# Score products of even and odd heads, alternating in one block behind both decay products

## The reference

```python
# for each step t
m_new = maximum(f + m, i);  f_stab = exp(f + m - m_new);  i_stab = exp(i - m_new)
C = f_stab * C + i_stab * outer(v, k);   n = f_stab * n + i_stab * k
y = sigmoid(o) * (C @ q) / maximum(abs(n . q), 1)
# layer 2: rms norm, then (silu(xn @ w_gate) * (xn @ w_val)) @ w_out     (320 -> 1536 -> 320)
# layer 3: g = h+ + alpha * h-  with h = x @ w_in;  g @ w_out2           (320 -> 2048 -> 320)
```

## Time and profile before

| | us |
|---|---|
| median of 3 runs | 541.23 (541.06 to 547.64) |
| span of the profiled execution | 539.5 |
| TensorE (PE) busy in it | 509.5 (94%) |
| VectorE (DVE) busy | 365.5 (68%) |
| ScalarE (ACT) busy | 203.3 (38%) |
| GpSimd (POOL) busy | 233.1 (43%) |

### The profile page before, as it was taken

The page is one execution under the profiler, slowest core; times in us unless marked ns, Lnnn a source line. Parts: engine busy times, 40 slices in busy tenths (PEclk is TensorE's granted clock), DMA queues, the critical chain, the costliest instruction groups (busy, mean ns, idle before and its releaser), DMA issues.

```text
span 539.5 us, 9907 instructions
## 1 busy us (share of the span) xinstructions
PE 509.5 (94%) x3113; PEld 485.2 (90%) x3113; DVE 365.5 (68%) x710; ACT 203.3 (38%) x508; POOL 233.1 (43%) x250
## 2 busy tenths in 40 slices
PE   5889888999999999999999999999999999998996
PEld 4778788998999999998999899999899899997996
DVE  7634589557899847346899848444999842228885
ACT  1322244434453532324453432324453432235452
POOL 3520066552564723423464723424374632223764
PEclk9755599999999999999899999999999999999999
DMA  7633742122333394000343477000333420003553
GB/s 129 162 63 49 148 134 78 50 70 47 73 111 107 83 143 68 1 1 24 66 124 88 105 119 95 0 0 0 76 108 106 103 73 2 0 1 77 129 140 97
DMA packets 80725, 41.14 MB, mean 76 GB/s; under 512 B 51548, under 2 KB 80684, under 8 KB 80684
## 3 DMA queue, kind: packets, MB, share of 16 engines
q1 hardware_dynamic: 80684, 40.65, 33.7%
HBM read 38.67 MB, written 1.97 MB: 75 GB/s over the span
## 4 chain that ended last, share of the span: by engine, by line
PE 41%; issue 25%; DVE 12%; POOL 12%; DMA 5%; ACT 2%; SPq 2%; POOLq 0%; DVEq 0%; ACTq 0%
PE bank L955 21%; PE bank L963 7%; POOL w L825 5%; POOL hidT L833 4%; PE bank L966 3%; PE bank L909 2%; PE bank L921 2%; DMA shared<-in_moe_w_in 2%; POOL decay_rhs L800 2%; DVE win L708 2%; DMA shared<-in_moe_w_out 1%; DVE u L738 1%; DMA shared<-in_moe_w_gate 1%; PE bank L915 1%; SPq L340 1%
## 5 line engine op out<-in xcount | busy, mean ns | idle before, releaser
L833 POOL TENSOR_TENSOR hidT<-hid,hidT 128x384 fp32r<-128x384 f32 x112 | 117.8, 1052 | 240.3 <-ACT hidT L494 238.9
L494 ACT CAST hidT<-hid 128x384 fp32r<-128x384 f32 x112 | 57.5, 513 | 142.7 <-DVE hid L721 86.1
L955 PE MATMUL bank<-x2T,win 128*128 128x384 f32 x512 | 103.2, 346 | 1.2 <-ACT x2T L535 0.7
L955 PEld LDWEIGHTS bank<-x2T,win 128*128 128x128 f32 x512 | 90.4, 194 | 2.1 <-issue 0.9
L955 PE MATMUL bank<-xT,wg 128*128 128x384 f32 x384 | 77.5, 344 | 5.0 <-DVE u L715 4.2
L715 DVE SCALAR_TENSOR_TENSOR u<-th,bank 128x384 f32<-128x384 f32 x48 | 26.6, 553 | 78.6 <-ACT th L516 75.8
L955 PE MATMUL bank<-xT,wv 128*128 128x384 f32 x384 | 76.1, 341 | 0.0
L963 PE MATMUL bank<-w,hidT 128*128 128x320 f32 x384 | 69.5, 316 | 4.7 <-POOL w L825 4.6
L955 PEld LDWEIGHTS bank<-xT,wg 128*128 128x128 f32 x384 | 66.5, 191 | 7.0 <-issue 4.8
L955 PEld LDWEIGHTS bank<-xT,wv 128*128 128x128 f32 x384 | 68.2, 191 | 0.5
L963 PEld LDWEIGHTS bank<-w,hidT 128*128 128x128 f32 x384 | 58.5, 188 | 9.4 <-POOL w L825 6.9
(11 more groups left out here) (127 smaller groups left out, 706.2 us busy)
## 6 DMA issues: line engine op xcount, KB each, us to landing
shared<-in_moe_w_out SPq DMA_DIRECT2D x38, 320.0 KB, 5.3
shared<-in_moe_w_in SPq DMA_DIRECT2D x34, 256.0 KB
shared<-in_moe_w_in SPq DMA_DIRECT2D x34, 128.0 KB
q_in<-in_q SPq DMA_DIRECT2D x12, 160.0 KB, 4.5
k_in<-in_k SPq DMA_DIRECT2D x12, 160.0 KB, 4.8
v_in<-in_v SPq DMA_DIRECT2D x12, 160.0 KB, 4.6
o_in<-in_o_gate SPq DMA_DIRECT2D x12, 160.0 KB, 4.3
shared<-in_moe_w_gate SPq DMA_DIRECT2D x6, 256.0 KB
```

The costliest lines, as they stand in the source:

```text
L494: a.copy(hidT[:, i % NH, 0], hid[:, i % 2]).then_inc(s_hid_hi, 1)
L833: gp.tensor_tensor(hidT[:, i % NH, 1], hid[:, i % 2], hidT[:, i % NH, 0].bitcast(F32), ALU.subtract).then_inc(s_hid_lo, 1)
L955: last = te.matmul(dst, w[:, blk, col:col + P], x[:, part, xb, :], start=(n == 0), stop=(n == len(terms) - 1))
```

## The change

On TensorE alone, S0 issues nothing any more, and S1 issues the score products of all eight heads, alternating between an even head (rows 0 to 39) and an odd one (rows 64 to 103). The first count of `s_S_mm` comes with the last even product, the second with the last odd one. VectorE, ScalarE and GpSimd keep their steps where they were, VectorE's wait and product at S0 among them.

```diff
                 elif what in ("S0", "S1"):
-                    half = int(what[1])
+                    if what == "S0":
+                        return
                     pe.wait_ge(s_qT, n + 1)
                     pe.wait_ge(s_kT, n + 1)
-                    if half:
-                        pe.wait_ge(s_dx, 2 * n + 1)
-                    for c in range(4):
-                        r = HP * half
-                        last = te.matmul(A[1 - half][:, c * CH:(c + 1) * CH], kT[r:r + D, c, :], qT[r:r + D, c, :], start=True, stop=True)
-                    last.then_inc(s_S_mm, 1)
+                    pe.wait_ge(s_dx, 2 * n + 1)
+                    for c in range(PAIRS):
+                        for half in range(2):
+                            r = HP * half
+                            last = te.matmul(A[1 - half][:, c * CH:(c + 1) * CH], kT[r:r + D, c, :], qT[r:r + D, c, :], start=True, stop=True)
+                            if c == PAIRS - 1:
+                                last.then_inc(s_S_mm, 1)
```

## The result

| | before | changed |
|---|---|---|
| median of 4 runs, us | 541.14 | 568.73 |
| all runs | 536.56 to 547.64 | 564.52 to 570.97 |
| span of the profiled execution | 539.5 | 567.4 |
| mean granted clock in it | 0.953 | 0.915 |

The ratio is 1.0515, with a 95% interval of 1.0465 to 1.0564. Executions of one kernel lie up to 3% apart here, and the ratios in this text compare each kernel's faster executions alone, so they need not be the quotients of the medians beside them. A difference under some 1% is not resolved by so few executions.

A forecast was written before the change was run, and what follows sets the result against it. PE (TensorE) was taken as the bound, 94% busy with no hole beside feed-forward work. Terms -1.1 + 11.4 + 9.1 + 0.6 + 1.3 = +21.3 us on a 539.5 span gave 560.8, median 562.5, range 549 to 572.

The forecast's parts named there:

- the hold-back of VectorE's queue: VectorE's work behind its S0 wait is held until the S1 block ends: +11.4 us in group 1, +9.1 in group 2.
- Switches, -0.38 a group: On PE, one score block instead of two pays the change to 40-row products and back once: -0.38 us a group.
- Pace inside the block, taken as serial: In the score block, weight loads follow one another, sixteen records at 0.11 us each, so alternation gains nothing.
- rival 1: In the score block, both halves' loads and products run side by side: +9.4 us, 550.6 in all; chance 0.32.
- Group 0 covered: Behind group 0's block, PE needs nothing held back in time to wait: only the gain, -0.4 us, three times.
- Group 1: Behind group 1's block, PE waits for hidT 11 and reaches the second x2T late: +3.8 us, three times, +11.4.
- T: The moment when PE is through with the score block and would start its next step.
- Group 2: Behind group 2's block, out2-5 waits for w_out2's low half and intra comes 3.0 us late: three times, +9.1.
- Clock, +1.3: Behind group 1, a stretch at 0.50 clock comes in the third tile too: +1.3 us.
- rival 2: 0.50 clock follows each of PE's six waits in groups 1 and 2: +7.8 us, 570.3 in all; chance 0.13.
- Prologue: +0.6 forecast: In the prologue, inter needs a pT that starts when the block is almost done: +0.2 us a group, +0.6.
- Rival 3: DVE's late work catches up before PE wants it, so no hold-back: 525.8, or 537.8 with serial loads; chance 0.05.

The follow-up runs named there:

- e3: Kernel before with one wait changed: at S0 VectorE waits for the group's second score count instead of the first; 575.7 us against 542.4.
- e2: Changed kernel with the block's four even heads first and the four odd ones behind, no alternation; 567.2 us against 540.7 for the kernel before.
- e7: Kernel before with the change made in group 1 of each tile only; 559.5 us (548.0 to 563.4) against 542.4.
- e8: Kernel before with the change made in group 2 of each tile only; 553.4 us against 542.4.
- e4: Changed kernel with the alternating block of eight heads issued at S0 and nothing at S1; 541.3 us against 540.7 for the kernel before.
- e5: Changed kernel plus 24 unread filler products behind the score block of groups 1 and 2; 562.0 us against 540.7 for the kernel before.
- e9: Changed kernel with the block at S0, plus 20 unread filler products behind inter of group 1; 540.4 us against 541.1 for the kernel before.
- e10: Changed kernel with the block at S0 and VectorE's second w_in piece behind its copy at x2; 532.0 us against 541.1 for the kernel before.
- e11: Changed kernel with the block at S0, VectorE's second w_in piece behind its x2 copy, and 10 filler products; 535.2 us against 541.1 for before.
- e1: Changed kernel with VectorE's wait and first pT product moved from S0 to S1, next to the second; 539.9 us against 540.7 for before.
- e6: Kernel before with the change made in group 0 of each tile only; 535.1 us against 542.4.
- e12: Kernel before with only VectorE's part of the second w_in piece moved behind its copy at x2; 535.0 us against 541.1.

## Why the prediction came out as it did

The sign and the cause, the hold-back of VectorE's queue at groups 1 and 2, were right: 562.5 forecast, 568.7 measured, inside 549 to 572. That the size came so near was luck. The pace inside the block was priced 11.9 us too high (562.5 against 550.6), the clock some 15 us too low, and 5.3 us at the loop's second pass had no term at all.

**Switches, -0.38 a group: part of more, not measured alone.** Removing S0 gave 1.2 to 1.3 us of PE where nothing waited, which is the whole 1.27 of rows 3, switches and records.

**Pace inside the block, taken as serial: wrong.** Sixteen alternating records start within 1.16 - 0.27 = 0.89 us, 0.056 a record. The two halves run side by side, loads too, which was rival 1. This step failed: "I take nothing, since the pace is the load's in the two rows that I have". That a load sets the pace of a block on the same rows says nothing about two loads on different rows, and no row of before had such a pair. What the Trainium skill (TensorEngine Tiling, Key Properties) states for rival 1, that different tiles load weights and multiply in parallel, was borne out by the 1.16 us of sixteen records, and should have weighed more than an extrapolation from rows of another kind. Rival 1's own figure, 550.6, would still have missed by 18 us.

**Group 0 covered: right.** No wait (228.60 to 229.69), and the change in that group alone is a gain.

**Group 1: right in place and size.** Forecast: PE held until T + 2.7, second x2T at T + 7.9. Measured: T = 253.93, out1-11 at T + 2.9, DVE's copy done at 261.96, T + 8.0. (7.9 less 3.76 is 4.1, not the 4.2 of the text; three groups make that 0.2 us.) But the steps between run at 0.50 and fill that time, so the late transpose shows as clock and hardly as a wait.

**Group 2: right in cause, wrong in two terms.** out2-5 was forecast at T + 2.8 and came at T + 3.05, because pT starts 0.26 us behind the block rather than 0.05 to 0.16. The gain of S0 was forecast as lost by 0.4 us; 1.06 was lost, to GpSimd's low half of w_out2 piece 3. I had looked at the weights of in6 and not at the step directly behind S0.

**Clock, +1.3: the term that was mis-sized.** It was some +16. I counted one more stretch of 3.4 us, though my own steps put PE still for 2.7 us at six places; rival 2 (0.13) named just this. Measured are 0.50 stretches of 13.7, 13.7 and 3.4 us behind group 1 and 6.8, 6.8 and 3.4 behind group 2. A forecast with side-by-side halves and this clock, 550.6 - 1.3 + 16.1, gives 565.4, and with the 5.3 us at the loop's turn 570.7, 2 us over the 568.7: the late x2T is in it twice, in rival 1's +3.0 a tile and in the 16.1.

**Prologue: +0.6 forecast, -3.8 in the trace**, for which rival 1 had -4.0.

**Rival 3** fell with e3: the wait alone, without any change of TensorE, costs 33 us.

## What to carry to other kernels

When work moves back in one engine's queue, leave no other engine's wait for it at the old place: a consumer that waits early in a strict queue holds back all its later work, and the price is paid where the producer needs that work right behind the moved step. Group 0, where it needs it late, gained; groups 1 and 2, where the next step had to wait 2.9 us, lost: +17 and +11 us when changed alone. Price a stand-still of TensorE of 2 us or more with the slow clock behind it: the six waits of the changed kernel cost 17.5 us and the slow steps behind them 16.1. And before a step moves forward, read when each of its inputs is ready in the trace at hand: the exponential of D0 in group 2, 1.6 to 1.9 us behind S0, was there to be read.

## What was not expected of the hardware

**Score products on the two row halves overlap fully, weight loads included**: 16 records of 40 x 128 by 128 in 1.16 us against 8 in 1.16; grouped by half they overlap in part (1.64 to the next step against 1.09).

**How much slow clock follows a wait is not a fixed price here.** Behind the 24 waits of 2.2 to 3.0 us at an out step (changed kernel, e2, e3, e7, e8) 0.50 was granted every time, for 3.4 to 13.7 us, and for the same 2.87 us wait in e3 once 3.4 and once 13.7. Behind the six of 2.1 to 2.2 us at x2T (e4, e5) it came five times, behind the ten of 1.9 to 2.0 us at S0 of group 2 (e4, e9, e10, e11) six times, and in e1 a wait of 1.5 us was followed by 10.2 us of it and two of 1.7 us by none. There is one trace for each kernel, so no rule is drawn from this.

**A stand-still at the loop's turn comes and goes with the kernel.** PE's first gate step of the loop's second pass waits for nothing that the profile shows:

```profile
332.75 2.92 PE L957 MATMUL bank<-xT,wg 128*128 128x384 f32 x8 [4.08 <-issue]
```

with another 1.3 us of slow clock behind it. It is 3.7 to 4.2 us in the traces of the changed kernel, e1, e2, e6, e7, e8, e11 and e12, 2.0 and 2.7 in e5 and e9, and absent in before, e3, e4 and e10. The page's count of instruction-queue packets goes with it: 28 or 29 where it is there (28 in the changed kernel), 19 where it is not. The name of these packets suggests that instructions are being fetched, which no run shows; with one trace for each kernel, whether the stand-still belongs to the kernel or to the execution stays open too. It is 5.3 of the 27.9 us between the two profiled spans, and it blurs all differences of that size here.
